# Splitting the last head's output and routing, loading an expert's rows in chunks, and moving two side jobs

## The reference

```python
def _attn_ref(q, k, v):                      # 2 x 8 heads, 1152 rows, 64 wide
    q_pool = q.reshape(B, H, S // 2, 2, D).mean(axis=3)     # 576 pooled queries
    scores = q_pool @ k.transpose(0, 1, 3, 2) / sqrt(D)
    attn = exp(scores - max)
    attn = attn / (attn.sum(-1) + 1e-09)
    return attn @ v

def _moe_ref(x, w_gate, w1, w2, capacity):   # 1152 tokens, 512 wide, 8 experts, 1024 hidden, capacity 288
    logits = x @ w_gate
    expert_idx = argmax(logits)
    gate_w = softmax(logits)[expert_idx]
    # token i goes to the next free slot of its expert, if one is left
    disp[e, counts[e]] = x[i]
    y = relu(disp @ w1) @ w2
    out[i] = gate_w[i] * y[expert_idx[i], pos[i]]

def _moe2_ref(x, w_gate, w1, w2):            # dense: every token through all 8 experts
    P = exp(x @ w_gate - max)
    for _ in range(8): P /= P.sum(1) + 1e-09; P /= P.sum(0) + 1e-09; P *= N / E
    out = sum over e of P[:, e] * (relu(x @ w1[e]) @ w2[e])
```

## Time and profile before

| | |
|---|---|
| median of 3 runs | 1342.04 us (1341.78 to 1343.69) |
| profiled execution, its own time | 1340.81 us |
| span of the profile | 1339.1 us |
| TensorE busy | 1296.7 us, 97% |
| VectorE, ScalarE, GpSimd busy | 508.0, 505.7, 502.9 us, 38% each |
| mean granted TensorE clock | 0.989 |
| chain that ended last | TensorE 91%, VectorE 3%, issue 1%, ScalarE 1%, DMA 1%, GpSimd 1% |

### The profile page before, as it was taken

How to read it: one execution, slowest core, us unless ns; L and a number is a source line. 1 busy time by engine, 2 the same in 40 slices (tenths; PEclk the granted TensorE clock), 3 DMA queues, 4 the chain that set the end, 5 groups by cost and what they waited for, 6 DMA issues and landing times.

```text
span 1339.1 us, 20887 instructions
## 1 busy us (share of the span) xinstructions
PE 1296.7 (97%) x7688; PEld 1213.4 (91%) x7688; DVE 508.0 (38%) x1313; ACT 505.7 (38%) x1031; POOL 502.9 (38%) x423
## 2 busy tenths in 40 slices
PE   7989999968999999999999999999999999999998
PEld 6989999967999999898999999999999999999997
DVE  8979999962222222145222222222222222222221
ACT  6757777764665454113113113113113113113110
POOL 6265557519888677004204104104105005005100
PEclk9989999988999999999999999999999999999999
DMA  4932223127566644001101101101101102100000
GB/s 135 281 109 90 89 90 121 63 92 249 154 175 202 193 147 158 32 0 63 64 1 64 63 0 63 63 0 63 63 0 69 57 0 78 47 0 0 23 24 18
DMA packets 63072, 107.23 MB, mean 80 GB/s; under 512 B 6598, under 2 KB 21190, under 8 KB 63008
## 3 DMA queue, kind: packets, MB, share of 16 engines
q1 hardware_dynamic: 58416, 96.99, 21.7%
q10 hardware_dynamic: 2816, 5.01, 1.8%
q0 software_dynamic: 1776, 4.37, 0.9%
HBM read 94.92 MB, written 11.81 MB: 80 GB/s over the span
## 4 chain that ended last, share of the span: by engine, by line
PE 91%; DVE 3%; issue 1%; ACT 1%; DMA 1%; POOL 1%; POOLq 0%; DVEq 0%; ACTq 0%
PE psum L1279 36%; PE psum L1292 29%; PE psum L1311 8%; PE psum L1149 6%; PE psum L1139 5%; PE psum L1164 5%; PE psum L1182 1%; DMA raw<-in_moe_w_dram 1%; POOL wsplit L479 1%; DVE raw L772 1%; PE psum L1268 1%; DVE acts L781 1%; DVE small L772 0%; ACT acts L564 0%; ACT raw L571 0%
## 5 line engine op out<-in xcount | busy, mean ns | idle before, releaser
L1279 PE MATMUL psum<-acts,wsplit 128*128 128x384 f32 (+1 forms) x3072 | 515.4, 328 | 0.0
L1279 PEld LDWEIGHTS psum<-acts,wsplit 128*128 128x128 f32 x3072 | 509.3, 189 | 1.8
L1292 PE MATMUL psum<-wsplit,acts 128*128 128x512 f32 x1728 | 397.3, 390 | 0.0
L1292 PEld LDWEIGHTS psum<-wsplit,acts 128*128 128x128 f32 x1728 | 323.7, 188 | 66.0
L479 POOL TENSOR_TENSOR wsplit<-raw,wsplit 128x512 fp32r<-128x512 f32 x128 | 162.7, 1295 | 492.1 <-ACT wsplit L564 492.1
L686 ACT ACTIVATE acts<-psum 128x384 fp32r<-128x384 f32 (+1 forms) x256 | 120.5, 471 | 560.9 <-PE psum L1279 560.8
L997 DVE SCALAR_TENSOR_TENSOR acts<-psum,acts 128x384 fp32r<-128x384 f32 (+1 forms) x256 | 136.1, 533 | 359.2 <-ACT acts L686 359.0
L484 POOL TENSOR_TENSOR wsplit<-raw,wsplit 128x512 fp32r<-128x512 f32 x128 | 161.3, 1301 | 110.8 <-ACT wsplit L564 110.8
L564 ACT ACTIVATE wsplit<-raw 128x512 fp32r<-128x512 f32 (+1 forms) x259 | 155.3, 623 | 85.2 <-PE psum L1292 75.0
L564 ACT ACTIVATE acts<-psum 128x384 fp32r<-128x384 f32 (+2 forms) x304 | 123.1, 448 | 121.4 <-PE psum L1311 55.5
L1106 DVE SCALAR_TENSOR_TENSOR x<-psum,pr,x 128x512 f32<-128x512 f32 x63 | 47.3, 751 | 293.1 <-PE psum L1292 293.1
(11 more groups left out here) (136 smaller groups left out, 605.6 us busy)
## 6 DMA issues: line engine op xcount, KB each, us to landing
raw<-in_moe_w_dram SPq DMA_DIRECT2D x64, 1024.0 KB, 5.2
raw<-in_k_dram SPq DMA_DIRECT2D x15, 576.0 KB, 5.8
small<-in_q_dram SPq DMA_DIRECT2D x15, 576.0 KB, 3.8
raw<-in_v_dram SPq DMA_DIRECT2D x16, 288.0 KB, 4.1
slots_in<-zero SPq DMA_DIRECT2D x1, 4608.0 KB, 19.3
x<-slots_in ACTq DMA_DIRECT2D x7, 576.0 KB, 4.9
out_dram<-zero SPq DMA_DIRECT2D x1, 2304.0 KB, 28.0
x<-slots_in ACTq DMA_DIRECT2D x1, 432.0 KB, 4.0
```

What stands on the lines that cost most here:

```text
L1279: last = mm(psum[:, f % HBANKS, 0:w], w1s[a][:, c, f * P:(f + 1) * P], src[z][:, c, cols], start=(c == 0 and (a, z) == (0, 0)), stop=(c == ...
L1292: last = mm(psum[:, bank, :], hs[a][:, f, t0:t0 + P], w2s[z][:, f, :], start=(i == 0), stop=(i == 3 * FC - 1))
```

## The change

Five edits come together.

1. **Last head in two parts.** Batch 1's tiles form two groups, tiles 0 and 1 and tiles 2 to 4 (`GROUPS`). In head 15 all 18 steps of r = 0 are done by tile 3. Its r = 1 steps are broken twice: after 6 the output of tiles 0 and 1 is turned, after 13 the slots of that group are counted. The output of tiles 2 to 4 is turned at the end into a bank of its own (`BTURN2`). VectorE goes through the routing once for each group. `exp_gate(1)` stands on ScalarE between the two copies `evac_ot`. ScalarE scales all five tiles.
2. **First expert's rows in four chunks.** ScalarE issues chunks 0 and 2, SyncE 1 and 3. The hidden sums of f = 0 to 3 stay open in their four banks and grow by one chunk c at a time as it comes.
3. **Two row buffers.** `drow` has two halves; the rows of expert e + 2 are issued while expert e is at work, those of expert 1 right behind chunks 0 and 2.
4. **Clearing in pieces.** `slots_in` is cleared in three pieces after the loads of heads 5 to 7, `out` in three after heads 9 to 11, `owners` after head 12.
5. **The guard on ScalarE.** The addition of 1e-9 to the row sums becomes an activation (`Identity` with a bias), after the first of the three copies of tile 4; VectorE keeps the reciprocal.

```diff
-            sp.wait_ge(consts, 5)
-            sp.dma_start(slots_in.rearrange("(p a) (b c) -> p (a b) c", p=P, c=P),
-                         zero[:, :].unsqueeze(1).broadcast_to([P, E * CAP // P * DC, P])).then_inc(zeroed, 16)
-            sp.dma_start(out.rearrange("(p a) (b c) -> p (a b) c", p=P, c=P),
-                         zero[:, :].unsqueeze(1).broadcast_to([P, NT * DC, P])).then_inc(out_cleared, 16)
+            def clear(to, rows, i, n, done):
+                part = to[i * rows // n:(i + 1) * rows // n, :].rearrange("(p a) (b c) -> p (a b) c", p=P, c=P)
+                sp.dma_start(part, zero[:, :].unsqueeze(1).broadcast_to([P, rows // n // P * DC, P])).then_inc(done, 16)
...
             for g in range(4, G):
                 load_head(g)
+                if 5 <= g < 8:
+                    clear(slots_in, E * CAP, g - 5, 3, zeroed)
+                if 9 <= g < 12:
+                    clear(out, N, g - 9, 3, out_cleared)
...
-            sp.wait_ge(d0_loaded[1], 16)
+            sp.wait_ge(scattered, 16 * RT)
+            for c in (1, 3):
+                sp.dma_start(drow[0][:, :, c * P:(c + 1) * P],
+                             slots_in[0:CAP, c * P:(c + 1) * P].rearrange("(t p) d -> p t d", p=SR))\
+                  .then_inc(d0_loaded[c], 16)
+            sp.wait_ge(d0_loaded[3], 16)
             load_w2(0, 0, 1)
...
+            def row_sums(g):
+                if not is_first(g):
+                    act.wait_ge(den_done, g)
+                act.wait_ge(exp_done, QT * (g + 1))
+                nc.scalar.activation(rden[:, :], sums[:, g % 2, :], ACT.Identity, bias=eps[:, 0:1]).then_inc(sum_done, 1)
...
                     for c in range(NC):
                         p_hi(g, v, t, c)
+                        if c == 0 and t == QT - 1:
+                            if first:
+                                act.wait_ge(consts, 21)
+                            row_sums(g)
...
             evac_ot(G - 1, 0)
+            exp_gate(1)
             evac_ot(G - 1, 1)
+            scale_rows(1)
+            exp_gate(2)
+            scale_rows(2)
...
             act.wait_ge(scattered, 16 * RT)
-            load_rows(0)
+            for c in (0, 2):
+                act.dma_start(drow[0][:, :, c * P:(c + 1) * P],
+                              slots_in[0:CAP, c * P:(c + 1) * P].rearrange("(t p) d -> p t d", p=SR))\
+                   .then_inc(d0_loaded[c], 16)
+            load_rows(1)
...
             LV = G - 1
-            values(G - 1, LV, 1, 0, VSTEPS)
-
-            turn_out(G - 1)
+            values(G - 1, LV, 1, 0, 6)
+            turn_out(G - 1, 0, 2)
+            values(G - 1, LV, 1, 6, 13)
+            prefix(1)
+            values(G - 1, LV, 1, 13, VSTEPS)
+            turn_out(G - 1, 2, QT, BTURN2)
...
             def expert1(e):
                 last = e == E - 1
-                for f in range(FC):
-                    if FC * e + f >= HBANKS:
-                        pe.wait_ge(h_done, FC * e + f - HBANKS + 1)
+                opening = HBANKS if e == 0 else 0
+                if e == 0:
+                    turn_rows(0, 0)
+                for c in range(DC if e == 0 else 0):
+                    if c < DC - 1:
+                        turn_rows(0, c + 1)
+                    for f in range(opening):
+                        hidden(0, f, dts, slice(0, CAP), CAP, range(c, c + 1), dt_done if f == 0 else None, 0)
+                for f in range(opening, FC):
+                    pe.wait_ge(h_done, FC * e + f - HBANKS + 1)
                     hidden(e, f, dts, slice(0, CAP), CAP, range(DC), dt_done if f == 0 else None, DC * e)
```

More of the change, by code:

```diff
@@ L234, in build_attention_moe_moe @@
         yx_done = sem("yx_done")
-        d0_loaded = [sem(f"d0_loaded{i}") for i in (0, 1)]
+        d0_loaded = [sem(f"d0_loaded{c}") for c in range(DC)]
         dt_ready = sem("dt_ready")
@@ L658, in lt_evac @@
                                      ACT.Copy).then_inc(lt_done, 1)
-            exp_gate(1)
-            for t in range(ACT_ROWS):
-                scale_rows(t)
             for f in range(FC):
@@ L668, in load_rows @@
             def load_rows(e):
[L670 to L677 removed]
+                act.dma_start(drow[e % 2], slots_in[e * CAP:(e + 1) * CAP, :].rearrange("(t p) d -> p t d", p=SR))\
                    .then_inc(d_loaded, 16)
@@ L701, in expert1 @@
                 last = e == E - 1
-                if not last:
-                    load_rows(e + 1)
                 if e:
@@ new lines, in turned, with scale_logits @@
+            def turned(a, z, t0, t1, bank):
+                return psum[:, bank, t0 * FD:t1 * FD].rearrange("p (t d) -> p t d", d=FD)[:, :, a:z]
+            def scale_logits(g, t0=0, t1=QT, bank=BTURN, turn=0):
+                dve.wait_ge(den_done, g + 1)
+                dve.wait_ge(misc_ready, g + 1 + turn)
+                nc.vector.tensor_tensor(lgh[:, t0:t1, g, :], turned(DH, FD, t0, t1, bank),
+                                        den[:, t0:t1].unsqueeze(2).broadcast_to([P, t1 - t0, E]),
@@ L820, in head @@
                             move_scores(*ahead(g, v, t, 2), c)
-                        if t == 0 and not first:
-                            row_sums(g - 1, 1 - v % 2, c)
+                        if t == 0 and c == 1 and not first:
+                            row_sums(g - 1)
                     if t == TURN and not first:
@@ L846, in head @@
                                                 ALU.subtract).then_inc(wg_split, 1)
-                    if last and t == QT - 1:
+                    if last and t == TURN:
                         add_heads(part[:, :, :], NH, G - 1)
@@ L1180, in turn_out @@
                     prefix(0)
-                for t in range(QT):
-                    last = mm(psum[:, BTURN, t * FD:(t + 1) * FD], ot[:, t * P:(t + 1) * P],
-                              gfold[:, bass.ds(g, 1), :].rearrange("p g c -> p (g c)"), start=True, stop=True)
+                for t in range(t0, t1):
+                    last = mm(psum[:, bank, t * FD:(t + 1) * FD], ot[:, t * P:(t + 1) * P],
+                              gfold[:, g, :], start=True, stop=True)
                 last.then_inc(misc_ready, 1)
             BESIDE = {0: (0, 9), 1: (9, VSTEPS), 2: (0, 8), 3: (8, 11), 4: (11, VSTEPS)}
+            LAST_BESIDE = {2: (0, 8), 3: (8, VSTEPS)}
             def beside(g, v, t):
-                if t >= 2:
+                if t >= 2 and is_last(g):
+                    if t in LAST_BESIDE:
+                        values(g, v, 0, *LAST_BESIDE[t])
+                elif t >= 2:
                     values(g, v, 0, *BESIDE[t])
@@ L1255, in totals @@
                 last.then_inc(tot_ready, 1)
[L1257 removed]
+            prefix(2)
             totals()
             def turn_rows(e, c):
[L1261 to L1265 removed]
+                if e == 0:
+                    pe.wait_ge(d0_loaded[c], 16)
+                else:
+                    if c == 0:
+                        pe.wait_ge(d_loaded, 16 * e)
                     pe.wait_ge(dt_done, DC * e + c)
@@ L1334, in expert1 @@
                     project_t(e, c, lambda: between(c))
-            for c in range(DC):
-                turn_rows(0, c)
             for e in range(E):
```

186 lines of the change are left out of this document (81 added, 105 removed).

## The result

| | before | after |
|---|---|---|
| median | 1341.91 us (1340.52 to 1343.69, 4 executions) | 1326.76 us (1326.58, 1326.73 and 1326.80, and a fourth of 2605.9) |
| profiled execution, its own time | 1340.81 | 1326.58 |
| span of the profile | 1339.1 | 1324.8 |
| mean granted clock | 0.989 | 0.993 |

The ratio is 0.9886, with a 95% interval of 0.9867 to 0.9905. The kernel is faster by 15.15 us, more than the range of the prediction took in: its direction was right and its size too small by 4.4 us.

What follows compares the result with a forecast made beforehand. TensorE was taken to set the pace, VectorE close behind. Terms 6.87 + 0.86 + 1.13 + 0.7 + 0 + 1.2 = 10.8 us off the profiled 1340.81 gave 1330.0, plus 1.2 for the median: 1331.2; range 1328.0 to 1335.0.

Steps and rivals of the forecast that it cites:

- Clearing in pieces: Head 3: loads no longer queue behind SyncE's clearing, so the head falls from 23.32 to 16.45 us, a gain of 6.87.
- rival (c): Heads 5 to 7: clearing pieces delay keys and make GpSimd late; 1337 us at 2 us each; chance 0.04 with (e).
- (e): Rival: TensorE's slack is given up elsewhere and head 3 keeps its stall; 1338 us; chance 0.04 together with rival (c).
- The two cancel; I take 0: Guard, steady heads: VectorE's relief and ScalarE's added operation offset each other; 0 us, with 1.5 either way.
- The excess of heads 2, 4 and 11: Heads with the guard's worst times: moving it to ScalarE gains 0.86, 1.13 and 0.7 us, 2.7 in all.
- Head 4: Its length over a steady head, 17.58 against 16.45 us, was put down to the slow guard; gain 1.13 us.
- Last head in two parts: Head 15: second turn 1.7 us later, but last scatter ends at 299.6 against 301.20; SyncE's two chunks gain 1.6 us.
- Only then does it issue chunks 0 and 2: Handover: ScalarE issues its chunks after its roundings end at 302.8, so the first chunk leaves 0.2 us later.
- The split over two queues: First expert's chunk loads: two queues save only issue time, half of 0.87 us; the sum takes nothing for it.
- The term of 1.2: Handover to the first expert: 0.2 us for the hidden sums plus 1.0 of the 1.19 us stall at 326.60.
- Rival (d): ScalarE's guard needs another table than the exponential: two loads a head, 37 us, time 1368 us; chance 0.03.
- Rival (a): Handover pays in full, 2.7 for 1.2 us, and the guard nets 1 more: 1328.7 us; chance 0.11.

Runs made afterwards that it cites:

- e1_clear: Kernel before with only the clearing in pieces: median 1334.72 us, ratio to before 0.9948.
- e8_guard_twice: Changed kernel with the guard operation done twice on ScalarE in each head, the first result unused: median 1329.31 us, ratio to before 0.9916.
- e2_guard: Kernel before with only the guard moved to ScalarE: executions of 1338.08, 1339.77, 1430.64 and 1604.07 us, no ratio given.
- e10_one_part: Changed kernel with the last head's output turned and routed in one part, ScalarE scaling all five tiles: median 1328.71 us, ratio to before 0.9896.
- e5_late_issue: Changed kernel with ScalarE waiting for all twelve weight roundings before issuing chunks 0 and 2: median 1326.90 us, ratio to before 0.9896.
- e12_one_queue: Changed kernel with all four chunks issued by ScalarE, none by SyncE: median 1325.94 us, ratio to before 0.9874.
- e7: Changed kernel with all four chunks turned before the first hidden matmul, open sums kept: median 1325.99 us, ratio to before 0.9889.
- e14: Changed kernel with all four chunks issued by ScalarE and all turned before the first hidden matmul: median 1327.45 us, ratio to before 0.9897.
- e4: Changed kernel with the guard back on VectorE in a form that also writes an accumulator: median 1326.78 us, ratio to before 0.9891.
- e13: Changed kernel run and profiled again without any edit: median 1327.08 us, ratio to before 0.9892.
- e9: Changed kernel with the guard back on VectorE in its plain form: median 1331.66 us, ratio to before 0.9913.
- e3: Kernel before with only the edits of the last head and the first expert: median 1337.35 us, ratio to before 0.9966.
- e6: Changed kernel with expert 1's rows issued behind the second chunk's copy: median 1328.86 us, ratio to before 0.9908.
- e11: Changed kernel with all chunks turned first and each hidden sum made in one go, none left open: median 1327.75 us, ratio to before 0.9883.

## Why the prediction was right, and where it failed

**Clearing in pieces: right.** 7.02 measured for 6.87, and e1_clear shows the mechanism alone. GpSimd waits for TensorE again (6.66 to 6.74 us in heads 4 to 8), and none of heads 5 to 7 lost anything, so rival (c) is out, and with it (e).

**The guard: the step that failed is "The two cancel; I take 0".** The excess of heads 2, 4 and 11 was forecast at 2.69 and measured at 2.89 (1.06 + 1.28 + 0.55). But ScalarE's loss of up to 0.1 us a head is nothing in the heads (e8_guard_twice: it starts with the second operation), and VectorE's gain is 0.19 a steady head: 0.76 + 0.39 + 0.74 = 1.9 us that was taken as 0. That is most of the 2.5 by which attention was missed. Another 0.28 lies ahead of the first milestone and is within what two profiles of the changed kernel differ by; the remaining 0.35 is in the terms for heads 2, 3, 4 and 11. The error is in the reading of the earlier trace rows: the median, 383 ns, was taken as 0.4 us of VectorE's work with 0.1 to 0.2 to gain, and then it was set off against a ScalarE cost bounded by adding its duration to the chain in the earlier trace rows. The chain has a gap before the second copy, which the rows of its start would have shown, and 383 for a minimum of 166 was VectorE standing still, in 12 of the 16 heads of before.

**Head 4: the sum right, the reason wrong.** Its 1.13 was put down to the guard's worst case. In e1_clear the guard stays on VectorE and head 4 falls to 16.49 all the same; in e2_guard the stall stays and head 4 falls to 16.28. It took both: the stall shifted head 4 so that its guard met the start of a GpSimd subtraction (1446 ns), and without the stall it meets the end of one (410 ns). So either edit gives this term, and only once. The excess of head 2 is the guard's alone (e2_guard: 1.06).

**Last head in two parts: right to 0.6 us at every step**, and worth 1.0 us in the end (e10_one_part).

**The chunks: "Only then does it issue chunks 0 and 2" failed.** The issue came at 300.9 on the old scale and not at 302.8, three roundings ahead of its turn. The first hidden matmul was 27.02 - 24.56 = 2.46 us sooner, not 1.55. e5_late_issue prices the missed step at 0.3 to 0.4 us in the end. The split over two queues, priced at nothing, cost 0.7 to 1.0 us at the first hidden matmul (e12_one_queue), about what the early issue gained there (0.7).

The term of 1.2 came out at 1.63, 0.4 too small, and its two parts were sized the wrong way round, which is luck. Forecast were 0.2 for the hidden sums, because ScalarE was thought to bind before and after, and 1.0 for the stall. Measured are 1.16 at the first `project_t` matmul (42.13 before, 40.97 after) and 0.49 from the stall (1.19 before, 0.70 after). The timeline of before shows why the 0.2 was wrong:

```profile
308.46 15.08 PE L1279 MATMUL psum<-acts,wsplit 128*128 128x288 f32 x96
```

All 96 hidden matmuls stand in one run, so the fifth sum did not wait for ScalarE before; TensorE, on its low clock, was itself the bound there. After, it waited 0.17 us: ScalarE took the first sum out 0.9 us sooner and had become level with TensorE.

**The rest.** Rival (d) is out: the only table load of the changed kernel is the one at its start, and the guard takes 291 ns. Rival (a) was the nearest in kind, the guard netting more and the handover paying more, but it was priced at 1 and 1.5 us instead of 2.5 and 0.4. The median's distance from its profile, 1.2, was carried over as a constant; it was 0.2 after. This 1.0 us is smaller than the spread of either kernel's executions (before: 1338.4 to 1345.59 us in all that were run). Together 2.5 + 0.4 + 0.5 + 1.0 = 4.4 us: 1331.2 instead of 1326.76.

## What to carry to other kernels

When a small operation shows a median far over its minimum and a worst case of several times that (166/383/1446 ns), price what its engine loses standing still in every repetition, not only in the worst ones, and try another form of the same operation before another engine: here that alone gave the same. Before you charge an inserted operation to a chain, look for the gap inside the chain; one operation fits in it and a second does not. And where TensorE resumes behind a long wait on a low clock, take what the clock took out of a difference before you credit an edit with it: e7 came 2.1 us sooner at `project_t`, e12 1.3 and the two together only 1.6, and the clock alone took 1.0, 1.6 and 2.4 us in them, for 2.7 in the changed kernel.

## What the runs showed of the hardware that was not expected

- A DMA issue on ScalarE did not wait for the operations ahead of it in its list: it stood at 288.84 us with three roundings of 0.61 us starting at 288.88, 289.40 and 289.92. With a wait put in (e5) it stood at 290.47.
- With four loads issued on one queue the first was turned 2.3 us after its issue (e12, e14); with the same four on two queues at once, 3.0 to 3.3 us (ten profiles).
- Behind the wait of some 10 us at the handover, the low clock took between 1.4 and 2.9 us in kernels with the same tail (lowest in e4, highest in e13); what sets the moment at which it ends stays open.
- An addition to five numbers on VectorE took from 161 ns (e9) to 1446 ns (before), by nothing but the moment at which it met a GpSimd subtraction of 1.43 us.
- In 7 of the 16 profiles, with the same instructions at that place, TensorE runs for some 3 us of the second mixture at a granted clock down to 0.50, behind 18 small matmuls for the gate logits. Twelve matmuls there take 3.69 us instead of 2.38. A window of e7_turn_first (columns as in the earlier trace rows) shows it:

```profile
553.00:555.00 2.00, 2.00 (x8) 1.80 (x8) 0.00 (x0) 0.08 (x1) 0.00 (x0) 0.50 0.00 0
```

and that of the changed kernel, at the same work, does not:

```profile
553.00:555.00 2.00, 2.00 (x15) 1.98 (x15) 0.46 (x2) 0.00 (x0) 0.00 (x0) 1.00 0.00 0
```

TensorE is busy throughout in both. The stretch is in the profiles of e2, e3, e4, e6, e7, e9 and e11 and in no other, so it belongs to no one edit; what brings it about stays open. It alone sets two single profiles some 1.3 us apart (the means from proj to the end with and without it).
